# Moving preparation, a second q and a buffer wait at the start of an attention and MoE kernel on one core

## The reference

```python
scores = scale * np.matmul(q, k.transpose(0, 1, 3, 2))
x = (log1p(abs(i - j)) / log1p(max(i, 1)))[..., None]
bias = np.maximum(x @ w1 + b1, 0.0) @ w2          # 32 hidden units, 8 heads
attn = softmax(scores + bias)
attn_out = np.matmul(attn, v)                     # -> x of 2304 tokens x 512
gate = 1.0 / (1.0 + np.exp(-(x @ w_gate)))
out = (gate * (x @ w_val)) @ w_out                # d_ff 1536
```

## Time and profile before

| what | us |
|---|---|
| median of 3 runs (lowest to highest) | 807.1 (806.58 to 808.11) |
| the profiled execution, its own time | 807.83 |
| its span (first to last instruction) | 805.9 |
| TensorE busy in it | 772.3 |
| VectorE busy | 349.4 |
| ScalarE busy | 344.6 |
| GpSimd busy | 194.8 |

### The profile page before, as it was taken

How to read it: one execution, slowest core, us unless ns; L and a number is a source line. 1 busy time by engine, 2 the same in 40 slices (tenths; PEclk the granted TensorE clock), 3 DMA queues, 4 the chain that set the end, 5 groups by cost and what they waited for, 6 DMA issues and landing times.

```text
span 805.9 us, 13830 instructions
## 1 busy us (share of the span) xinstructions
PE 772.3 (96%) x5296; PEld 640.5 (79%) x5296; DVE 349.4 (43%) x845; ACT 344.6 (43%) x684; POOL 194.8 (24%) x363
## 2 busy tenths in 40 slices
PE   5776999999999999999799999999999999999998
PEld 2334777777777777789789998999899899989996
DVE  6995777777777777622421230222022212211220
ACT  6885676776676766632321220222122112212210
POOL 0001677557554547768100000000000000000000
PEclk9998999999999999999899999999999999999999
DMA  5779234242333231223312000100200020000001
GB/s 128 160 184 208 67 86 116 68 113 66 100 78 80 68 99 48 68 77 90 130 53 66 0 1 27 53 1 1 76 3 1 14 66 1 1 26 14 1 1 39
DMA packets 86336, 49.92 MB, mean 62 GB/s; under 512 B 60160, under 2 KB 79744, under 8 KB 86272
## 3 DMA queue, kind: packets, MB, share of 16 engines
q1 hardware_dynamic: 86272, 49.05, 23.3%
HBM read 28.98 MB, written 9.44 MB: 48 GB/s over the span
## 4 chain that ended last, share of the span: by engine, by line
PE 85%; DMA 4%; ACT 4%; SPq 2%; POOL 2%; issue 2%; DVE 1%; DVEq 0%; POOLq 0%; ACTq 0%
PE f_ps L1049 18%; PE g_ps L997 17%; PE u_ps L997 16%; PE v_ps L977 11%; PE so_ps L912 8%; PE ty_ps L925 4%; PE tx_ps L938 3%; DMA bias<-last_rows 2%; PE so_ps L907 2%; SPq L384 1%; ACT feats L574 1%; PE tx_ps L955 1%; POOL w L525 1%; PE ty_ps L880 1%; PE so_ps L857 1%
## 5 line engine op out<-in xcount | busy, mean ns | idle before, releaser
L997 PE MATMUL g_ps<-x_h,w 128*128 128x384 f32 x576 | 148.0, 338 | 4.1 <-DVE hid L826 4.1
L997 PE MATMUL u_ps<-x_h,w 128*128 128x384 f32 x576 | 146.5, 335 | 0.0
L826 DVE TENSOR_TENSOR hid<-u_ps,sig 128x384 f32<-128x384 f32 x72 | 40.1, 557 | 240.6 <-PE u_ps L997 240.6
L615 ACT ACTIVATE probs<-neg_scores,neg_max 128x576 f32<-128x576 f32 x144 | 111.1, 772 | 62.3 <-DVE neg_max L750 62.3
L508 POOL TENSOR_SCALAR probs<-probs,recip 128x512 f32<-128x512 f32 x128 | 88.7, 693 | 167.0 <-DVE recip L770 167.0
L997 PEld LDWEIGHTS g_ps<-x_h,w 128*128 128x128 f32 x576 | 105.0, 190 | 5.2 <-DVE hid L826 4.5
L997 PEld LDWEIGHTS u_ps<-x_h,w 128*128 128x128 f32 x576 | 104.3, 188 | 0.5 <-issue 0.5
L681 ACT ACTIVATE h_h<-hid 128x384 fp32r<-128x384 f32 x72 | 37.8, 526 | 149.8 <-DVE hid L826 149.8
L997 PE MATMUL g_ps<-x_l,w 128*128 128x384 f32 x288 | 97.1, 337 | 0.0
L997 PE MATMUL u_ps<-x_l,w 128*128 128x384 f32 x288 | 96.3, 334 | 0.0
L750 DVE CUSTOM_DVE_ANT_0 neg_scores<-so_ps,bias 128x576 f32<-128x576 f32 x128 | 91.9, 756 | 5.6 <-DMA bias<-last_rows 5.2
(11 more groups left out here) (88 smaller groups left out, 1134.4 us busy)
## 6 DMA issues: line engine op xcount, KB each, us to landing
bias<-bias_rows SPq DMA_DIRECT2D x12, 576.0 KB, 6.1
x_raw<-attn_transposed SPq DMA_DIRECT2D x6, 768.0 KB, 4.6
out<-out_sb SPq DMA_DIRECT2D x18, 256.0 KB, 2.0
q_raw<-in_q SPq DMA_DIRECT2D x32, 128.0 KB, 2.5
k_raw<-in_k SPq DMA_DIRECT2D x32, 128.0 KB, 2.5
v_main<-in_v SPq DMA_DIRECT2D x32, 128.0 KB, 2.3
w_raw<-in_w_gate SPq DMA_DIRECT2D x12, 256.0 KB, 2.8
w_raw<-in_w_val SPq DMA_DIRECT2D x12, 256.0 KB, 2.9
```

Source lines behind the costliest of these rows:

```text
L615: nc.scalar.activation(probs[s % RING][:, place, :], neg_scores[:, place, :], ACT.Exp, bias=neg_max[:, stat(s, place)], scale=-1.0, accum_ ...
L826: nc.vector.tensor_tensor(hid[f % 2][:, :], u_ps[f % 3][:, 0:CH], sig[f % 2][:, :], ALU.mult).then_inc(gated, 1)
L997: last = nc.tensor.matmul(bank[f % 3][:, 0:CH], w[:, f, part, i, t, :], x[:, t, :], start=m == 0, stop=m == len(terms) - 1)
```

## The change

- Pair 0's preparation is spread: q at unit 6, tails at unit 8, k at unit 10 on PE; ACT's high part one unit later each, DVE's low part three units later.
- Pair 1's q is turned and split in step 2 of attention, in the same PSUM tile as all others; pair 2's q is loaded in step 3 in place of ahead of duo 11's store.
- The fourth row buffer lies over the third probabilities tile (`probs2`), first written in step 2, in place of `neg_scores`. The first shift waits for duos 0 to 7 only.
- The three small constants are issued by ScalarE's queue, `inv_pos` first.
- PE multiplies the identity by itself six times (128x192) ahead of its wait for the constants, once GpSimd has made it (`ident_ready`, 3).

```diff
+WARM_UP = 6
 PREP_UNIT = 6
-SECOND_UNIT = 18
+TAILS_UNIT = 8
+KEYS_UNIT = 10
...
-        probs = [sb(f"probs{i}", [P, 2, S]) for i in range(RING)]
-        prob_tails = [sb(f"prob_tails{i}", [P, 2, REM]) for i in range(RING)]
+        probs = [sb(f"probs{i}", [P, 2, S]) for i in range(RING - 1)]
         with ExitStack() as bias_only:
             last_rows = sb("last_rows", [P, 2, S], F32, bias_only)
+        probs.append(sb(f"probs{RING - 1}", [P, 2, S]))
+        prob_tails = [sb(f"prob_tails{i}", [P, 2, REM]) for i in range(RING)]
         neg_scores = sb("neg_scores", [P, 2, S])
...
         # sync
             sp.dma_start(log_win[:, :], log_dist).then_inc(log_win_in, 16)
-            sp.dma_start(hidden_cols[:, :], hidden_wb).then_inc(hidden_in, 16)
-            sp.dma_start(inv_pos[:, :], inv_log_pos).then_inc(inv_pos_in, 16)
-            sp.dma_start(w2_rows[:, :], w2_sets).then_inc(w2_in, 16)
...
-                if d == SECOND_UNIT // 2 + 2:
-                    sp.wait_ge(q_turned, 2)
-                    load_q(2)
                 store_bias(d)
...
                 if s in (0, 2):
                     load_v(s // 2)
+                if s == 3:
+                    sp.wait_ge(q_turned, 2)
+                    load_q(2)
...
         # scalar
+            act.dma_start(inv_pos[:, :], inv_log_pos).then_inc(inv_pos_in, 16)
+            act.dma_start(hidden_cols[:, :], hidden_wb).then_inc(hidden_in, 16)
+            act.dma_start(w2_rows[:, :], w2_sets).then_inc(w2_in, 16)
             act.wait_ge(zero_ready, 1)
...
-                if u == PREP_UNIT:
+                if u == PREP_UNIT + 1:
                     high_q(0)
+                if u == TAILS_UNIT + 1:
                     high_tails(0)
+                if u == KEYS_UNIT + 1:
                     high_k(0)
-                if u == SECOND_UNIT:
-                    high_q(1)
...
+                if s == 2:
+                    high_q(1)
...
         # vector, shift
-                        to = ROW_STEP if s == 0 and d < ROW_BUFS - 1 else DUOS
+                        to = ROW_STEP if s == 0 else DUOS
...
-                if u == PREP_UNIT + 1:
+                if u == PREP_UNIT + 3:
                     low_q(0)
+                if u == TAILS_UNIT + 3:
                     low_tails(0)
+                if u == KEYS_UNIT + 3:
                     low_k(0)
-                if u == SECOND_UNIT + 1:
-                    low_q(1)
...
                     move_b(s - LAG)
+                if s == 2:
+                    low_q(1)
...
         # tensor
+            pe.wait_ge(ident_ready, 3)
+            for n in range(WARM_UP):
+                nc.tensor.matmul(v_ps[:, 0:P + REM], ident, ident_wide[:, :], start=True, stop=True)
             pe.wait_ge(hidden_in, 16)
...
                     turn_q(0)
+                if u == TAILS_UNIT:
                     turn_tails(0)
+                if u == KEYS_UNIT:
                     turn_k(0)
-                if u == SECOND_UNIT:
-                    turn_q(1)
...
                     transpose_b(c)
+                    if s == 2:
+                        turn_q(1)
                     if m == 4 and pair + 2 < PAIRS:
                         turn_q(pair + 2)
                     transpose_a(c, tails_of)
```

More of the change, by code:

```diff
@@ L280, in score_ps @@
             return so_ps[:, at:at + 2, 0:HALF]
-        def q_turned_ps(pair):
-            return tx_ps[:, 0:NT * P] if pair == 1 else v_ps[:, 0:NT * P]
         def set_rows(j):
@@ L589, in high_q @@
                     act.wait_ge(scored, SPP * (pair - 1) - 1)
-                nc.scalar.activation(qk_h[pair % 2][:, Q_MAIN:], q_turned_ps(pair), ACT.Copy).then_inc(q_high, 1)
+                nc.scalar.activation(qk_h[pair % 2][:, Q_MAIN:], v_ps[:, 0:NT * P], ACT.Copy).then_inc(q_high, 1)
             def high_k(pair):
@@ L724, in low_q @@
                 dve.wait_ge(q_high, pair + 1)
-                nc.vector.tensor_tensor(qk_l[pair % 2][:, Q_MAIN:], q_turned_ps(pair), plain(qk_h[pair % 2][:, Q_MAIN:]),
+                nc.vector.tensor_tensor(qk_l[pair % 2][:, Q_MAIN:], v_ps[:, 0:NT * P], plain(qk_h[pair % 2][:, Q_MAIN:]),
                                         ALU.subtract).then_inc(q_low, 1)
@@ L865, in turn_q @@
                     pe.wait_ge(x_ready[1], pair - 2)
-                elif pair == 2:
-                    pe.wait_ge(q_low, 1)
-                to = q_turned_ps(pair)
+                elif pair >= 1:
+                    pe.wait_ge(q_low, pair)
+                to = v_ps[:, 0:NT * P]
                 for t in range(NT):
@@ L934, in transpose_a @@
                 else:
-                    pe.wait_ge(q_low, 2)
                     pe.wait_ge(tails_low, 2)
```

## The result

The changed kernel takes 801.4 us (median of 6 runs, 799.04 to 802.29) against 807.1 before (806.58 to 808.11): ratio 0.9927, 95% interval 0.9915 to 0.9939, that is 5.9 us less by the ratio and 5.7 by the medians. The forecast was 802.1, range 799.9 to 805.0. The profiled execution took 801.9 (span 799.9; before 807.83 and 805.9 in the profiled one).

A forecast was written before the change was run, and what follows sets the result against it. Ahead of attention, VectorE's and ScalarE's pace bounds up to duo 9, then DMA engines draining bias stores. Terms 0.8 + 1.9 + 1.3 + 1.9 - 0.7 - 0.2 = 5.0 us gave 802.1 us, range 799.9 to 805.0.

The forecast's parts named there:

- What sets the end: Bias stage: engine pace up to duo 9, then DMA draining stores; small stores at 37.1 us, step-2 shift near 74.
- The start: Ahead of and in units 0 to 3: earlier high clock less a later unit 0, +0.8 us (-0.4 to +1.8).
- the constants: Start of the kernel: issued by ScalarE's queue, they come earlier, alone worth 0 to 0.9 us of issue time.
- The identity products: TensorE from 2.1 to 6.1 us: unit 0 0.45 us later, but up to 2.3 us won if the clock is high.
- Pair 0's preparation: Ahead of duo 8: spread, it costs 1.7 us instead of 3.6, a gain of 1.9 (0.4 to 2.1).
- Pair 2's q out of the stores: Full DMA stretch of bias stores: 256 KB less brings all later stores' landing 1.3 us earlier.
- The fourth row buffer: First shift no longer waits for duo 15; the wait moves to step 2, gaining 1.9 us.
- The costs behind: After step 2's wait: low clock slows TensorE in two steps, 0.7 us; pair 2's q late in step 4, 0.2.
- The slower rival: Pair 2's q over 5.2 us late blocks TensorE in step 4; 808.7 us if 6.8 late; late q's chance 0.05.

The follow-up runs named there:

- e3: Changed kernel with pair 0's q, tails and k all at unit 6 again, VectorE's part at unit 7: 803.76 us, ratio 0.9961.
- e4: Changed kernel with pair 1's q prepared at unit 18 again, VectorE's part at 19; pair 2's q still loaded in step 3: 802.33 us, ratio 0.9937.
- e10: Changed kernel with small-store duos last, v and first weights loaded early, pair 2's q in step 1, row buffers over other memory: 801.01 us, ratio 0.9918.
- e1: Changed kernel without the identity products: 801.01 us, ratio 0.9928.
- e2: Changed kernel without identity products and with the constants back on SyncE's queue: 801.07 us, ratio 0.9929.
- e5: Changed kernel with the fourth row buffer over neg_scores again, so the first shift waits for duo 15: 803.83 us, ratio 0.9956.
- e11: As e10, with the constants back on SyncE's queue and five identity products for six: 800.39 us, ratio 0.9913.
- e12: As e11, with pair 1's q prepared between the last bias unit and the first step, pair 2's q loaded in step 0: 799.83 us, ratio 0.9896.
- e7: Changed kernel with half of the sixteen small stores issued by GpSimd's queue: 803.53 us, ratio 0.9957.
- b1: Kernel before with the fourth row buffer alone, the first shift no longer waiting for duo 15: 806.12 us, ratio 0.9975.
- e6: As e4, with pair 2's q loaded ahead of duo 11's store again: 803.65 us, ratio 0.9951.
- the rerun: The changed kernel as it is, run again beside the first group of experiments: 801.62 us, ratio 0.9935.

## Why the prediction was right, and where it wasn't

**What sets the end.** Right. The small stores' beginning moved by 2.25 us (2.7 forecast), the shift of step 2 is held by the last store, and all behind it moved as one. The range and the sign followed from that. That what lies ahead of duo 8 counts is shown by e3's runs. That what lies behind is covered holds for the queue of stores (e4); but the chain from the last copy ends only 1.3 to 1.7 us ahead of the queue in the changed kernel (an estimate: 6.35 us from the first shift, as in e10, for the 7.66 and 8.04 that its two profiles show), and of a stall of 2.7 us some 0.9 to 1.9 came through.

**The start, +0.8 forecast.** Too high. It was 0.3 in the profile and nothing in the runs (e1, e2). The step that failed is the constants: priced from 0 to 0.9 us of gain, they cost 0.66 us at the first features (e1 against e2), because the bounds came from the issue order and left out that q and k would move up beside them. The Trainium skill (page "DMA: Bandwidth & Descriptors", section "Issuing engines are not separate DMA queues") speaks of saved issue time only; here it was a loss. The identity products ended at 6.34 (6.1 forecast), and in 3 of the 10 profiles that have them (e3, e5, e10) unit 0 ran at high clock and unit 5's copy came about 1.1 us earlier (16.4 to 16.5 against 17.5 to 17.9; e11 and e12, with earlier constants, left aside); in none of the 4 without. (In e7 a part of unit 0 did.) That points to their working sometimes, but 3 in 10 against 0 in 4 can be chance, and the spread without them is wide too: the records turned fast at 10.1, 11.4, 12.6 and 13.3 us in those 4. In e3 nothing of the gain was left at unit 17.

**Pair 0's preparation, +1.9.** The size is right (2.1 us undone alone, e3); its working holds for about half of it. From unit 5's copy to unit 17's it took 19.29 us for 21.25, which is 1.96; but in b1 and e3, which prepare pair 0 at once as well, it took 20.32 and 20.31. The other 0.9 the kernel before lost in a stretch of low clock right behind its stall, which neither of these two had. Against them the units gain 1.0 and not 1.9. The windows behind the stall, first of before, then of e3:

```profile
23.30:26.60 3.30, 3.01 (x31) 1.47 (x32) 2.46 (x6) 2.28 (x4) 0.00 (x0) 0.50 0.41 84
...
20.80:26.60 5.80, 4.71 (x64) 1.96 (x64) 5.80 (x13) 4.56 (x7) 0.00 (x0) 1.00 0.42 105
```

The prediction's 3.6 us for the preparation, read from units 5 to 8, holds this low clock: it is 2.65 in b1 and e3. What the prediction did not have is that in the profiles with the preparation spread SyncE issues the small stores faster, by 0.4 to 1.9 us. From unit 5's copy to duo 10's issue it took 32.9 to 33.8 us in the three profiles with the preparation at once, and 30.3 to 31.4 in the seven with it spread and the small stores in the middle: 2.6 us on the average.

**Pair 2's q out of the stores, +1.3.** Right. From duo 10's issue to the landing of the v load behind the last store it took 26.4 to 26.5 us in the three profiles that load this q among the stores (before, b1, e6), and 24.2 to 25.0 in the seven that don't (the changed kernel twice, e1 to e5); e6 against e4, which differ in this alone, gives 1.4. By the runs it is 1.1 to 1.3.

**The fourth row buffer, +1.9.** Right: 2.0 alone (b1), 1.7 undone (e5), and 1.4 to 2.0 in the profiles of the two. What it gives is the difference between two waits in one chain, not the idle time of 5.16 us that the profile shows at the first.

**The costs behind, -0.7 and -0.2.** The mechanism came (2.02 us idle, then clock 0.50 from 75.6 to 79 us), the cost did not: from the shift of step 2 to pair 1's scores it took 7.65 us, and 7.68 before. The prediction took TensorE for the bound of these steps at low clock. But in that stretch the kernel before has TensorE waiting for VectorE for 1.20 and 0.30 us, so a slower TensorE had room. e2 shows that the low clock is free there: its low clock was over at 74.1 us, the shift of step 2 came at 73.91, and the same stretch took it 7.74 us. And the kernel before had low clock too, but mostly ahead of the shift at 80.01: its 7.04 us between the first shift and that one are at low clock, where e10, with the clock high until 68.4 us, took 6.35. The windows (columns as above; 0.50 and 0.99 are the granted clock), first of before, then of e2's stretch:

```profile
74.50:81.20 6.70, 6.20 (x36) 5.25 (x37) 4.36 (x13) 3.60 (x11) 3.19 (x7) 0.50 1.03 184
...
73.90:81.60 7.70, 5.58 (x48) 4.71 (x46) 6.14 (x18) 5.69 (x13) 3.49 (x8) 0.99 0.67 159
```

Pair 2's q was in time.

**What the sum lacked.** SyncE took 0.96 us less for the small stores in this profile (0.37 in the rerun); part of that is spread, and part belongs to pair 0's preparation, as above. In the feed-forward part TensorE was busy for 443.4 of 450 us and not for all of it, and 0.57 was lost at the link to it. By the two profiles the landing of the v load moved by 5.1 us: 2.25 by the start of the small stores (2.7 forecast), 0.96 by their issue (0 forecast), 1.9 behind duo 10 (1.3). The moved wait then gave 1.5 (1.9), the costs behind nothing (0.9), and the link took 0.6. So the errors nearly cancel, which is luck in part: 5.0 forecast, 5.7 measured by the medians, 5.9 in the profiled executions.

**The slower rival** (pair 2's q late by more than 5.2 us) did not come: it was issued at 76.00, SyncE was not slowed (1.05 us for the two loads, 2.57 before), and TensorE did not wait. The loads landed in 2.6 us, the short end of the 2.5 to 5 allowed, 0.8 us ahead of their use.

## What to carry to other kernels

Find the queue that is full for longest and ask where it starts to be full: a stall ahead of that point counts in full, a stall behind it is free only until the chain of the compute engines ends later than the queue (2.7 us of stall in e4 passed that point). An idle time in front of a wait is not what its removal brings; the next wait in the same chain is, and only the difference between the two counts. And when a wait that covered a step goes, price the step again: what was free in step 2 of the changed kernel cost about a microsecond in e11 (9.42 us for 8.40 in e12).

One profile of the baseline is one sample. Two later profiles with the same preparation showed that 0.9 us of its stall was a low clock that does not always come.

## What was not expected of the hardware

A load of 1 KB took 3.5 to 3.8 us to land on SyncE's queue ahead of q and k, and 4.3 to 4.6 on ScalarE's, issued at the same time. Idle TensorE time of 2.09 us was followed by low clock in the profile of before and not in those of e3 and b1, at the same unit, though there the idle time was the same to 10 ns. And SyncE needed between 10.2 and 12.1 us for the same sixteen issues, all times over 11.4 in kernels that prepare pair 0 at once; most issues took 0.58 to 0.62 us, and up to two of the later fifteen 0.8 to 1.8.
